# First attended block of a two-layer kernel: loads on one queue, sums shared out anew, the left half split ahead

## The reference, cut to what matters

```python
k_p = k.reshape(B, H, Sp, pool, D).mean(axis=3)        # B=8 H=8 S=576 D=64, pool=8: Sp=72
v_p = v.reshape(B, H, Sp, pool, D).mean(axis=3)
scores = np.matmul(q, k_p.transpose(0, 1, 3, 2)) / np.sqrt(D)
attn = softmax(scores)
x = np.matmul(attn, v_p)                                # to 4608 rows of 512
h = x @ w_in;   x = (h * sigmoid(h)) @ w_out             # 512 -> 2048 -> 512
h = x @ w_in2;  out = (h * clip(h + 3, 0, 6) / 6) @ w_out2
```

## Time and profile before

| | us |
|---|---|
| median of 3 runs | 1722.51 (1721.97 to 1722.82) |
| the profiled execution, its own time | 1724.1 |
| its span | 1722.3 |
| busy: TensorE | 1684.0 (98%) |
| busy: VectorE, ScalarE, GpSimd | 1034.8, 725.6, 329.8 |

### The profile page before, as it was taken

One profiled execution on the slowest core, in us unless ns is written; L12 is line 12 of the kernel. 1 busy time (PEld: TensorE's weight loads), 2 busy tenths in 40 slices (PEclk: granted clock), 3 DMA queues, 4 the chain that ended last, 5 costly groups with the idle time before them and its releaser, 6 DMA issues.

```text
span 1722.3 us, 27457 instructions
## 1 busy us (share of the span) xinstructions
PE 1684.0 (98%) x11104; PEld 1511.6 (88%) x11104; DVE 1034.8 (60%) x1567; ACT 725.6 (42%) x1182; POOL 329.8 (19%) x431
## 2 busy tenths in 40 slices
PE   7789999999999999999999999999999999999999
PEld 6769888888989999999999899999998899999998
DVE  5757567556645655555555765555556766666664
ACT  3645555555454533333333444333344533333332
POOL 4176336434303500000005300000006200000000
PEclk9899999999999999999999999999999999999999
DMA  7233334333222322222223311111112322222221
GB/s 190 74 104 105 111 94 112 107 98 112 80 77 86 124 85 74 74 74 74 74 74 123 98 50 50 49 50 50 49 50 98 123 74 74 75 79 80 80 78 52
DMA packets 129838, 145.83 MB, mean 85 GB/s; under 512 B 47536, under 2 KB 74416, under 8 KB 129712
## 3 DMA queue, kind: packets, MB, share of 16 engines
q1 hardware_dynamic: 77888, 127.42, 22.6%
q10 hardware_dynamic: 51824, 16.65, 3.9%
HBM read 96.86 MB, written 47.19 MB: 84 GB/s over the span
## 4 chain that ended last, share of the span: by engine, by line
PE 89%; DVE 5%; ACT 2%; issue 1%; DMA 1%; POOL 1%; ACTq 0%; SPq 0%; DVEq 0%; POOLq 0%
PE zw L597 7%; PE zw L599 7%; PE zw L598 7%; PE acc L671 6%; PE xy L597 5%; PE xy L599 5%; PE xy L598 5%; PE acc L673 5%; PE acc L672 5%; PE acc L678 4%; PE acc L677 4%; PE acc L679 4%; PE att L679 4%; PE att L678 4%; PE att L677 4%; PE att L671 2%
## 5 line engine op out<-in xcount | busy, mean ns | idle before, releaser
L1161 DVE TENSOR_TENSOR g_lo<-g_raw,g_hi 128x1024 fp32r<-128x1024 f32 x144 | 196.7, 1368 | 7.8 <-ACT g_raw L877 7.8
L865 ACT COPY x_sum<-xy 128x256 f32<-128x256 f32 x144 | 52.5, 365 | 308.7 <-PE xy L599 308.5
L1128 DVE TENSOR_TENSOR x_sum<-xy,x_sum 128x256 f32<-128x256 f32 x144 | 60.5, 420 | 196.1 <-ACT x_sum L865 196.1
L597 PE MATMUL xy<-xr_hi,w1r_hi 128*128 128x256 f32 x576 | 167.4, 291 | 7.2 <-DVE xs_lo L1200 5.1
L671 PE MATMUL acc<-g_hi,w_hi 128*128 128x512 f32 x400 | 166.4, 416 | 0.0
L599 PE MATMUL xy<-xr_hi,w1r_lo 128*128 128x256 f32 x576 | 163.5, 284 | 0.0
L598 PE MATMUL xy<-xr_lo,w1r_hi 128*128 128x256 f32 x576 | 163.5, 284 | 0.0
L673 PE MATMUL acc<-g_hi,w_lo 128*128 128x512 f32 x400 | 156.9, 392 | 0.0
L672 PE MATMUL acc<-g_lo,w_hi 128*128 128x512 f32 x400 | 156.6, 392 | 0.0
L517 POOL TENSOR_TENSOR w_sum<-w_raw 128x256 f32<-128x256 f32 x16 | 16.1, 1006 | 727.2 <-DMA w_raw<-in_moe_w_in_dram 727.2
L1152 DVE TENSOR_TENSOR g_raw<-zw,x_sum 128x512 f32<-128x512 f32 x144 | 99.0, 688 | 92.2 <-PE zw L599 92.2
(11 more groups left out here) (184 smaller groups left out, 4842.2 us busy)
## 6 DMA issues: line engine op xcount, KB each, us to landing
partial<-y_stage SPq DMA_DIRECT2D x72, 256.0 KB, 2.0
y_part<-partial SPq DMA_DIRECT2D x18, 1024.0 KB, 5.9
x_raw<-first_layer_t SPq DMA_DIRECT2D x18, 1024.0 KB, 7.7
x_raw<-attended_t SPq DMA_DIRECT2D x10, 1024.0 KB, 8.1
first_layer_t<-y_stage SPq DMA_DIRECT2D x36, 256.0 KB, 2.0
out_dram<-y_stage SPq DMA_DIRECT2D x36, 256.0 KB, 2.0
w_raw<-in_moe_w_in_dram SPq DMA_DIRECT2D x16, 512.0 KB, 4.2
kv_stage<-in_v_dram SPq DMA_DIRECT2D x56, 144.0 KB
```

The lines of the kernel that those rows point to most:

```text
L597: nc.tensor.matmul(dst, s_hi[i], m_hi[i], start=first and i == 0, stop=False, skip_group_check=True)
L1161: nc.vector.tensor_tensor(g_lo[:, p], g_raw[:, p % 2], g_hi[:, p].bitcast(fp32), ALU.subtract)\
```

## The change

Nothing is left out of the computation. What is done otherwise, all before step 0 or inside it:

- SyncE issues all loads; queries 0 and 1 come behind the keys, and weight quarter 1 comes ahead of the keys of batch 1.
- TensorE turns the identity 56 times (`WARM`) before the first queries.
- GpSimd sums half of the values and half of the next keys (`first_pair`, three adds for two heads). The values of batch 0 go to spare room beside the weight sums (`first_value`). TensorE is left with `sum_v(2)`, `sum_v(3)`, `sum_k_next(2)` and `sum_k_next(3)`, the last inside `chunk_a(0, 0)`.
- The left half of x is rounded and split (`round_x_first`, start of `first_block`) ahead of the last tiles' copies; `chunk_a(0, 0)` waits for that, for its second product and for its third apart. The fifth tile has buffers of its own (`q_fifth`, `qt_fifth`), and its scores also move into `chunk_a(0, 0)`.
- ScalarE's order changes; `round_w2` moves to places 0, 1, 2, 3, 5, 6, 7, U, `split_w1(0, 2)` and `split_w1(0, 3)` to after places 1 and 3, `pt` and `pv` of the fifth tile one place later each.
- From w2 tile 2 on, loads and sums of batch 1's values go in turn with the w2 tiles, on SyncE and on GpSimd, and those values no longer wait for the fifth tile.

```diff
@@ -65,8 +65,8 @@
-PLAN_FIRST = {1: [("kt",), ("qt", 0)], 2: [("exp", -1, 0)], 3: [("norm", -1), ("s", 0)], 4: [("pt", -1), ("qt", 1)],
-              5: [("pv", -1), ("s", 1)], 6: [("qt", 2)], 7: [("s", 2)], U + 2: [("qt", 3)], U + 4: [("s", 3), ("exp", 0, 3)],
+PLAN_FIRST = {1: [("kt",), ("qt", 0)], 2: [("exp", -1, 0)], 3: [("norm", -1), ("s", 0)], 4: [("qt", 1)],
+              5: [("pt", -1), ("s", 1)], 6: [("pv", -1), ("qt", 2)], 7: [("s", 2)], U + 2: [("qt", 3)], U + 4: [("s", 3), ("exp", 0, 3)],
@@ -140,7 +140,8 @@
-W2_FIRST_AT = [3, 4, 5, 6, 7, U]
+W2_FIRST_AT = [0, 1, 2, 3, 5, 6, 7, U]
+WARM = 56
@@ -358,6 +362,11 @@
+        def first_value(h, heads=1):
+            at = h % GH * D
+            return w1_sum0[:SP, 2 + h // GH, 3, at:at + heads * D]
@@ -444,22 +453,23 @@
-            for c in (2, 3):
+            for c in range(FIRST):
...
-            sp.dma_start(q_first[:ROWS[FIRST], FIRST], q_rows(FIRST)).then_inc(first_q_loaded[FIRST], 16)
+            load_w1(0, 1)
...
-            sp.wait_ge(k_first_added, 3)
+            sp.wait_ge(first_added, 3)
...
-            for p in range(1, NPAIR):
-                load_w1(0, p)
+            sp.dma_start(q_fifth[:ROWS[FIRST]], q_rows(FIRST)).then_inc(first_q_loaded[FIRST], 16)
+            load_w1(0, 2)
+            load_w1(0, 3)
+            for i in range(2):
+                load_w2(0, i)
...
-            for i in range(2):
-                load_w2(0, i)
@@ -469,10 +479,13 @@
-            for f in range(2, NF):
+            load_w2(0, 2)
+            load_w2(0, 3)
+            for f in range(4, NF):
+                load_kv(f - 2)
...
-            for n in range(2, H):
-                load_kv(n)
+            load_kv(NF - 2)
+            load_kv(NF - 1)
@@ -535,7 +548,7 @@
-                    else:
+                    elif b > 1:
@@ -558,22 +571,37 @@
-            pair = k_first[:, 4:6]
+            def first_pair(n, src, dst):
+                nc.gpsimd.tensor_tensor(src[:, :, :4 * D], src[:, :, :4 * D], src[:, :, 4 * D:], ALU.add)\
+                    .then_inc(first_added, 1)
+                pool.wait_ge(first_added, 3 * n + 1)
+                nc.gpsimd.tensor_tensor(src[:, :, :2 * D], src[:, :, :2 * D], src[:, :, 2 * D:4 * D], ALU.add)\
+                    .then_inc(first_added, 1)
+                pool.wait_ge(first_added, 3 * n + 2)
+                nc.gpsimd.tensor_tensor(dst, src[:, :, :D], src[:, :, D:2 * D], ALU.add).then_inc(first_added, 1)
...
-            nc.gpsimd.tensor_tensor(pair[:, :, :4 * D], pair[:, :, :4 * D], pair[:, :, 4 * D:], ALU.add).then_inc(k_first_added, 1)
-            pool.wait_ge(k_first_added, 1)
-            nc.gpsimd.tensor_tensor(pair[:, :, :2 * D], pair[:, :, :2 * D], pair[:, :, 2 * D:4 * D], ALU.add)\
-                .then_inc(k_first_added, 1)
-            pool.wait_ge(k_first_added, 2)
-            nc.gpsimd.tensor_tensor(k_pool[:, 4:6], pair[:, :, :D], pair[:, :, D:2 * D], ALU.add).then_inc(k_first_added, 1)
-            for p in range(NPAIR):
-                sums(0, p)
-            for f in range(NF):
-                if f >= NF - 2:
-                    pool_head(f - (NF - 2))
+            first_pair(0, k_first[:, 4:6], k_pool[:, 4:6])
+            for j in range(2):
+                pool.wait_ge(v_loaded[j], 16)
+                first_pair(1 + j, v_first[:, 2 * j:2 * j + 2], first_value(2 * j, 2).rearrange("r (h d) -> r h d", d=D))
+            sums(0, 0)
+            sums(0, 1)
+            pool.wait_ge(kt_done, 1)
+            for j in range(2):
+                pool.wait_ge(k_next_loaded[j], 16)
+                first_pair(3 + j, k_first[:, 2 * j:2 * j + 2], k_pool[:, 2 * j:2 * j + 2])
+            sums(0, 2)
+            sums(0, 3)
+            split_w2(0, 0)
+            split_w2(0, 1)
+            for f in range(2, NF):
+                pool_head(f - 2)
...
-            for n in range(2, HEADS):
+            for n in range(NF - 2, HEADS):
@@ -631,7 +662,14 @@
+                if s == 0 and p == 0:
+                    sum_k_next(3)
+                    first_scores(FIRST)
+                if p == 0:
+                    pe.wait_ge(x_split, 4 * s + 2)
...
+                if s == 0 and p == 0:
+                    pe.wait_ge(x_split, 3)
@@ -802,40 +842,36 @@
 
             def attend_first():
                 pe.wait_ge(ident_ready, 2)
+                for i in range(WARM):
+                    nc.tensor.transpose(zw[1][:, :P], ident[:], ident[:])
                 first_queries(0)
+                pe.wait_ge(first_pooled, NK - 1)
+                pe.wait_ge(first_added, 3)
+                transpose_k(acc[1])
                 first_queries(1)
-                pe.wait_ge(first_pooled, NK - 1)
-                pe.wait_ge(k_first_added, 3)
-                transpose_k(acc[1])
-                first_queries(2)
                 pe.wait_ge(first_kt_copied, 2)
                 first_scores(0)
+                first_queries(2)
                 first_scores(1)
                 first_queries(3)
                 first_scores(2)
-                sum_v(0)
                 pe.wait_ge(first_s_read, 2)
                 first_scores(3)
-                sum_v(1)
+                sum_v(2)
                 first_turn(0)
-                sum_v(2)
                 sum_v(3)
                 first_turn(1)
                 pe.wait_ge(v_copied, 1)
+                pe.wait_ge(first_added, 9)
                 first_values(0)
-                pe.wait_ge(first_s_read, 2 * FIRST)
-                sum_k_next(0)
                 first_turn(2)
                 first_values(1)
-                sum_k_next(1)
-                sum_k_next(2)
                 first_turn(3)
                 first_values(2)
                 first_queries(FIRST)
-                sum_k_next(3)
                 first_values(3)
-                pe.wait_ge(first_x_copied, 3)
-                first_scores(FIRST)
+                pe.wait_ge(first_s_read, 2 * FIRST)
+                sum_k_next(2)
 
             attend_first()
             for s in range(STEPS):
@@ -918,6 +949,25 @@
+            def round_x_first():
+                act.wait_ge(first_x_copied, 2)
+                act.wait_ge(qt_done, FIRST)
+                nc.scalar.activation(xr_hi[:, :, :HB], x_raw[:, :, :HB], ACT.Copy).then_inc(x_rounded, 1)
+            def round_x_second():
+                act.wait_ge(pv_done, FIRST)
+                act.wait_ge(x_summed, 2)
+                nc.scalar.activation(xs_hi[:, 1], x_sum[:, 1], ACT.Copy).then_inc(x_rounded, 1)
+                nc.scalar.activation(xr_hi[:, :, HB:], x_raw[:, :, HB:], ACT.Copy).then_inc(x_rounded, 1)
+                act.wait_ge(x_summed, 3)
+                nc.scalar.activation(xs_hi[:, 0], x_sum[:, 0], ACT.Copy).then_inc(t3_rounded, 1)
+            def round_x_last():
+                act.wait_ge(x_summed, 4)
+                nc.scalar.activation(xs_hi[:, 2], x_sum[:, 0], ACT.Copy).then_inc(x_rounded, 1)
@@ -1047,39 +1096,37 @@
                         nc.scalar.copy(x_out[:, 2 * (c - 2):2 * (c - 1), :], src[:, 0:2]).then_inc(first_x_kept, 1)
 
                 copy_q(0)
-                copy_q(1)
                 act.wait_ge(kt_done, 1)
                 src = acc[1][:, :NK * SP].rearrange("p (j r) -> p j r", r=SP)
                 nc.scalar.copy(kt[:D, :, :SP], src[:D]).then_inc(first_kt_copied, 1)
                 nc.scalar.copy(kt[D:, :, SP:], src[D:]).then_inc(first_kt_copied, 1)
+                copy_q(1)
                 copy_q(2)
+                exp(0)
                 copy_q(3)
-                exp(0)
                 exp(1)
+                exp(2)
                 copy_p(0)
-                exp(2)
-                act.wait_ge(v_summed, 1)
-                nc.scalar.copy(v_pool[:], acc[1][:SP].rearrange("r (h d) -> r h d", d=D)).then_inc(v_copied, 1)
+                act.wait_ge(v_summed, 2)
+                nc.scalar.copy(first_value(GH, GH), acc[1][:SP, 2 * P:]).then_inc(v_copied, 1)
                 copy_p(1)
+                round_w1(0, 0)
+                exp(3)
                 copy_x(0)
-                exp(3)
+                round_w1(0, 1)
                 copy_p(2)
-                round_w1(0, 0)
                 copy_x(1)
                 copy_p(3)
+                round_x_first()
                 copy_x(2)
                 copy_q(FIRST)
                 copy_x(3)
-                for part in range(4):
-                    round_x(0, part)
-                    if part == 1:
-                        round_w1(0, 1)
-                act.wait_ge(k_next_summed, 1)
+                round_x_second()
+                act.wait_ge(k_next_summed, 2)
                 act.wait_ge(kt_done, 1)
-                nc.scalar.copy(k_pool[:], ab[0][:SP].rearrange("r (h d) -> r h d", d=D)).then_inc(k_next_copied, 1)
+                nc.scalar.copy(k_pool[:, GH:], ab[0][:SP, 2 * P:].rearrange("r (h d) -> r h d", d=D)).then_inc(k_next_copied, 1)
+                round_x_last()
                 round_w1(0, 2)
-                round_w2(0, 0)
```

(85 more changed lines are left out.)

15 lines of the change are left out of this document (5 added, 10 removed).

## The result

The changed kernel takes 1710.38 us (median of 4 runs, 1709.72 to 1712.23) against 1722.24 in the runs of the kernel before beside it: 0.9929 of it, 95% interval 0.9914 to 0.9944. It is faster, but by 11.9 us where 21.9 were predicted, and 1710.4 lies above the range's upper end of 1709.

The account below looks back on a forecast made before the run. TensorE was taken as the bound, busy nearly throughout, with gains possible only in the first 131.5 us. Terms 14.0 + 5.7 + 2.2 = 21.9 and 1.6 over the median, off 1724.1, gave 1700.6 us; range 1695 to 1709.

Parts of the forecast that it names:

- One queue: Start of the kernel: with all keys loaded ahead of all queries, the last keys land 2.5 us sooner, at 8.9.
- 56 turns: Start, on TensorE: identity turns end at about 10 us and bring scores 0.6 to 1 us sooner; first shift 12.8.
- Values of batch 1: At pv(0): values are ready 2.4 us ahead of the due time 87.4, so TensorE's 5.7 us wait goes.
- the slow stretch: Behind pv(0), 107 to 112 us at granted clock 0.50: goes with the wait for values, 2.2 us gained.
- The softmax: First block, VectorE: 15.8 us of work stay, idle time falls from 3.1 to 1.0, last norm ends at 29.6.
- From softmax to copied block: First block, last norm to copy_x(3): GpSimd's weight sums come last; copy_x(3) starts at 35.1 against 44.47, 9.4 us gained.
- Left half ahead: x sums and splits before step 0's products: last split at 43.1, first chain_u at 44.6 against 57.14, 12.5 us sooner.
- Step 0 up to `qt(1)`: VectorE is the bound; one split_w1 (2.15 us) leaves, 1.5 taken, so qt(1) is 14.0 us sooner, at 55.7.
- GpSimd is late for the first block: Rival: slow GpSimd sums or long identity turns put 4 to 5 us on copy_p(2) or keys; 1704 to 1707, chance 0.17.

Follow-up runs that it names:

- e3: Changed kernel with GpSimd's adds for next keys and weight quarters 2 and 3 on 4 columns only, plus 39 more identity turns on TensorE: 1703.41 us.

## Why the prediction was wrong

**Held.** *One queue*: taken 2.5, measured 2.3 (keys at 9.02, predicted 8.9). *56 turns*: predicted to end at about 10, ended at 10.1; first shift 13.19 for 12.8. *Values of batch 1*: 5.7 taken for the wait and 2.2 for the slow stretch. `pv(0)` gained 5.5 over `qt(1)`, step 1 another 1.8 over `pv(0)`; undoing that part alone cost 7.7 (7.1 by the ratios) against 7.9. In e3 `pv(0)` came at 88.30 and did not wait either, so this was not luck of a late first block. The wait of 3 to 4 us before `qt(1)` stayed, at 3.1.

**Failed.** The term of 14.0 us that the first block was to bring up to `qt(1)`; it brought 5.9. Four steps of it:

- *The softmax*, "gain of 5.7", last norm at 29.6: it ended at 31.76. The first shift was 0.4 late; the rest is VectorE's work: from there to the end it is busy for 17.9 us in place of 15.8, and rests 0.7 where 1.0 was taken. All four norms ran at about 1.12, for which the text named 0.7 us and did not take them; they cost 0.5 (4.47 us together, 4.01 before, where three and not two had run long). What the sum left unpriced were the four TENSOR_SCALARs of 8 columns: 3.30 us together, 1.24 before (records overlap a little, so the busy time grows by less than the two together). The trace of the kernel before had two of them at 0.56 and 0.34 beside GpSimd's adds, and two at 0.17.
- *From softmax to copied block*, where "GpSimd, not VectorE, is what comes last": ScalarE waited 0.34 us for a weight sum. What came last was TensorE: the turn of tile 3, the values of tiles 2 and 3, the fifth tile's queries and a sum, at half clock, put copy_x(3) at 38.21 for 35.1 and the first product at 41.43 for 35.5. Of copy_x(3)'s 3.1 us, 2.2 are the softmax's; from the last norm's end to it lie 6.4 us, and 4.7 in e3, where the clock held. My sum took this work at full clock. I had looked at the clock for the products behind a rest, not for the turns, which now stand behind short rests of 0.6 to 2.2 us.
- *Left half ahead*: the splits were taken at 1.22 + 0.95 and the x sums at their old pace. But the change itself moved GpSimd's adds there: two pairs of next keys, behind which quarters 2 and 3 end at 47.0 us, where before they had ended ahead of the x sums. So `xr_lo` started at 38.49 for 34.0 and the last split ended at 49.7 for 43.1. The prediction weighed VectorE's loss by the contention for the norms alone, at 0.7 us.
- *Step 0 up to `qt(1)`*, "I take 1.5": from the first `chain_u` to `qt(1)` it took 12.8 us, 12.5 before and 11.1 in the sum. The one `split_w1` left there ran beside a `split_w2` that the change had moved ahead (`w1s_lo` 2.03 us for 0.95), and VectorE waited 0.54 and 0.67 us for products that the slow clock had made late.

The lines of the last point, of VectorE and of GpSimd:

```profile
57.40 2.03 DVE L1296 TENSOR_TENSOR w1s_lo<-w_sum,w1s_hi 128x768 fp32r<-128x768 f32 x1
```

```profile
56.60 2.00 POOL L565 TENSOR_TENSOR w_lo<-y_stage,w_hi 128x512 fp32r<-128x512 f32 x1 [3.81 <-ACT w_hi L988]
```

*What the runs showed in their place.* In short, two engines ran slower than the sum had them: VectorE beside GpSimd's adds, and TensorE at half clock. With GpSimd's adds thinned and the clock held, the forecast's times came within 1 us and the kernel took 1703.4, of the 1700.6 predicted. So the order of events was right, and the durations of two engines were not. What was not foreseen at all is that two costs lie beside each other. The rival that came nearest, "GpSimd is late for the first block" (4 to 5 us), priced one of them, and its mechanism, weight sums that hold up ScalarE's queue, did not occur.

*Left over.* 2.8 us between 1703.4 and 1700.6. In the trace that kernel's span is 20.8 us shorter where the sum had 21.9. At `qt(1)` it is 14.3 us ahead of the kernel before (14.0 in the sum), at `pv(0)` 18.8 (19.7) and at step 1 20.8 (21.9), so this 1.1 is lost behind `qt(1)`, most of it ahead of `pv(0)`; why stays open. The other 1.6 are those that the prediction took off because the profiled execution of before lay over its median; the profiled run of this kernel, 1703.3, stands at its own median, and where the 1.6 went isn't settled. The same holds for the changed kernel: 8.5 of the 9.8 us missed are in the trace (21.9 for 13.4).

The Trainium skill ("GPSIMD Engine Reference", the hardware table) names the contention for VectorE instructions with two SBUF inputs or in a 2-port perf mode. The traces agree for the splits and sums, which have two inputs. The TENSOR_SCALAR has one, and took 1.16 us beside GpSimd's adds and 0.17 without; whether it runs in such a mode no trace shows.

## What to carry to other kernels

When work moves to an engine that shares something with the engine on the critical path, price every operation of that path in the new stretch at its slowed duration, the smallest included: one of 8 columns can last as long as the add that it meets. Read the granted clock of the stretch in front of the place where work becomes dense, and ask what short rests the change leaves there. When one suspected cost is removed and nothing moves, remove two together before the theory is dropped.
